# Attention of the next block set between the products of the feed forward

## The chip, the cores and the metric

The kernel runs on one core of one Trainium2 chip. Its time is device time in microseconds (us) of one execution, median of several. The engines are named PE (TensorE, matrix products; PEld is its loading of weights), DVE (VectorE), ACT (ScalarE), POOL (GpSimd) and SP (SyncE, which here only starts transfers). Each engine works through a queue of its own in order and waits on semaphores for the others.

## The reference

Three layers follow each other, all in float32.

```python
# 1: attention, batch 4, 8 heads, 576 positions, 64 wide
scores = scale * np.matmul(q, k.transpose(0, 1, 3, 2))
mask = (rel >= 0) & (rel < 64)            # a position sees itself and 63 before
attn = softmax(where(mask, scores, -1e9))
x = matmul(attn, v)                       # rearranged to (2304, 512)
# 2: feed forward, 512 -> 2048 -> 512
h = x @ w_in
g = h - np.tanh(h)
x2 = g @ w_out
# 3: eight experts, each token goes to the one with the largest cosine
logits = xn @ en.T / tau
expert_idx = np.argmax(logits, axis=1)
out[mask] = gate_w[mask, None] * (np.maximum(x2[mask] @ w1[e], 0.0) @ w2[e])
```

The products of layers 2 and 3 are made in three passes: each operand is split in a rounded part (high) and the rest (low), and high x high, high x low and low x high are added up in PSUM.

## The kernel before

**Attention** is a stage of its own at the start. Its unit of work is a *group*: for one pair of heads, three blocks of 64 positions (GB = 3). A batch has 12 groups (4 pairs of heads x 3 windows of 192 positions), so there are 48 (NG). The work on group g is spread over steps of a pipeline (`attention_step`); in step j

- PE transposes q and k of group j (`transpose_qk`, L1003), does the scores of j-1 (`score`, L1012), transposes the weights of j-5 (`transpose_p`, L1021) and multiplies those of j-7 by v (`attend`, L1032);
- DVE takes q (scaled) and k of group j out of PSUM (`evacuate`, L721 and L723), masks the scores of j-1 and finds their maximum (`mask_max`, L728), inverts the sums of j-3 (L749, L754) and copies v of group j-5 from the lower to the upper half of the partitions (`shift_v`, L738), since each block sees the one before it too;
- ACT does three exps for j-1 (`exp`, L536), copies the transposed weights of j-5 (`copy_pT`, L544) and the attended group j-7 (`copy_x`, L553, two copies of 64x192) into `xT`, which holds x of all tokens, transposed;
- POOL multiplies the weights of j-3 by the inverse sums (`normalise`, L416) and between that splits w_in (L428, L431) from a staging tile, a piece every third step;
- SP starts the loads of q, k and v, and one row block of w_in per batch.

**Feed forward** follows. A block is 384 tokens (TB), there are 6 (NBLK). For each of 16 chunks c of 128 hidden columns: PE makes the first product (12 matmuls of 384 columns, `first_product`) and the second product of chunk c-2 (9 matmuls of 512 columns, `second_product`), both through `products` (L1059 to L1061); ACT does tanh (L581), DVE h - tanh(h) (L796), ACT rounds it (L585), DVE makes its rest (L798). The second product adds up in three PSUM banks (`acc`); at c == 2 of the next block they are copied out, and at c = 3 to 11 the router of that block has its turn on PE, DVE and ACT (`after_block`: transposes of x2 at L1097, logits, choice of an expert, rank in its table); SP stores x2 and POOL scatters the slots. At c = 10 to 13 ACT and DVE split x of the next block, `xT` into `xh` and `xl` (`round_x` L571, `rest_x` L785). While the first block runs, POOL splits w_out (L478, L480), whose rows come in through the tile x2.

**Experts**: at the end the tables are planned, and 25 tiles of up to 128 tokens are gathered, put through two products with the expert's weights, and scattered. The first expert's weights are fetched once x of the last block has been split.

Both first stages run their middle part in loops with a register as counter (`attention`, `feed_forward`), with a first and a last part written out.

Of the kernel before, what the change touches and what calls it, by code (L numbers as in the profile page):

```python
# [6 lines left out]
F32R = mybir.dt.float32r  # L7
# [4 lines left out]
ds = bass.ds  # L12
# [5 lines left out]
HEAD = 9  # L18
# [16 lines left out]
def build(nc, q, k, v, w_in, w_out, emb, tau, w1, w2, out):  # L35
# [15 lines left out]
    NT = T // P  # L51

# [9 lines left out]
    with ExitStack() as ctx:  # L62
# [37 lines left out]
        changes = sb("changes", [P, NTILE + 1])  # L100

        phase1 = ctx.enter_context(ExitStack())
        xT = sb("xT", [P, NW, PAIRS, GT], scope=phase1)
        win_h = sb("win_h", [P, KC, F], F32R, phase1)
        win_l = sb("win_l", [P, KC, F], F32R, phase1)
        attn = ExitStack()

        vw = [sb(f"vw{i}", [P, NB + 1, 2, D], scope=attn) for i in range(PAIRS)]
        qbd = [sb(f"qbd{i}", [P, NB, 2, WINDOW], scope=attn) for i in range(2)]
        sm = [sb(f"sm{i}", [P, GB, P], scope=attn) for i in range(4)]  # L110
        pn = [sb(f"pn{i}", [P, GB, P], scope=attn) for i in range(4)]
# [3 lines left out]
        plain_ones = sb("plain_ones", [P, P], scope=attn)  # L115
        plain_tri = sb("plain_tri", [P, P], scope=attn)
# [5 lines left out]
        stage = sb("stage", [P, 2, F], scope=attn)  # L122

        kT = [sb(f"kT{i}", [P, NB + 1, WINDOW], scope=attn) for i in range(2)]
        qk = [sb(f"qk{i}", [P, NB, 2, D], scope=attn) for i in range(2)]
        attn.close()
        wout_h = sb("wout_h", [P, FC, DM], F32R, phase1)
        wout_l = sb("wout_l", [P, FC, DM], F32R, phase1)
        xh = sb("xh", [P, KC, 2, 2, GT], F32R, phase1)
        xl = sb("xl", [P, KC, 2, 2, GT], F32R, phase1)  # L130
        early = ExitStack()
# [3 lines left out]
        zrow = sb("zrow", [1, DM], scope=early)  # L135
        en1 = sb("en1", [E, 3], scope=early)
        enroot = sb("enroot", [E, 1], scope=early)
        early.close()
        gf_tile = sb("gf", [P, 2, TB], scope=phase1)
        gf = [gf_tile[:, i, :] for i in range(2)]  # L140
        gh = [sb(f"gh{i}", [P, TB], F32R, phase1) for i in range(2)]
        gl = [sb(f"gl{i}", [P, TB], F32R, phase1) for i in range(2)]
# [3 lines left out]
        x2T, junk = (xT[:].rearrange("p w k t -> p (w k t)")[:, i * BANK:(i + 1) * BANK] for i in (0, 1))  # L146
# [38 lines left out]
        first_loaded, v_shifted = sem("first_loaded"), sem("v_shifted")  # L185
        qk_loaded, v_loaded = sems("qk_loaded", 2), sems("v_loaded", PAIRS)
        win_loaded, win_split = sem("win_loaded"), sem("win_split")
        win_high = sem("win_high")
        qk_transposed, qk_evacuated = sem("qk_transposed"), sem("qk_evacuated")
        scored, maxed, exped = sem("scored"), sem("maxed"), sem("exped")  # L190
        sum_padded, inverted, normed = sem("sum_padded"), sem("inverted"), sem("normed")
        p_transposed, pT_copied, attended, x_copied = sem("p_transposed"), sem("pT_copied"), sem("attended"), sem("x_copied")
        wout_loaded = sems("wout_loaded", ST)
        wout_high, wout_split = sem("wout_high"), sem("wout_split")
        x_high, x_split = sem("x_high"), sem("x_split")
# [26 lines left out]
        psT, psS, psP, psO = ([grouped(2 * n + i) for i in range(2)] for n in range(4))  # L222
        psH = [banks[:, i, 0:TB] for i in (0, 1)]
        acc = [banks[:, 2 + i, :] for i in range(ST)]
        psX = banks[:, 5, :]
        psX_last = [banks[:, i, :] for i in (5, 2, 3)]
        psJ = banks[:, 0, :]
        psL = banks[:, 6, 0:ST * E].rearrange("p (s e) -> p s e", s=ST)
        psR = banks[:, 7, 0:ST * E].rearrange("p (s e) -> p s e", s=ST)
        psN = banks[:, 7, 0:E]  # L230
# [15 lines left out]
        def attention(eng, step):  # L246

            for j in range(HEAD):
                step(0, j)
            with eng.Fori(0, B - 1) as b:  # L250
                for j in range(HEAD, HEAD + GPB):
                    step(b, j)
            for j in range(HEAD, GPB + 7):
                step(B - 1, j)

        def feed_forward(eng, step):

            for c in range(FC):
                step(0, c)
            with eng.Fori(1, NBLK - 1) as n:  # L260
                for c in range(FC):
                    step(n, c)
            for c in range(FC):
                step(NBLK - 1, c)
# [28 lines left out]

        block = ctx.enter_context(nc.Block())

        @block.sync
        def _(sp):
            def load_qk(b, hp):
                i = hp % 2

                wait(sp, qk_transposed, 0 if isinstance(b, int) and PAIRS * b + hp < 2 else GPB * b + GP * (hp - 1))
                for blocks, to in ((q_blocks, qk[i][0:WINDOW]), (k_blocks, qk[i][WINDOW:P])):
                    for h in range(2):
                        sp.dma_start(to[:, :, h, :], blocks[:, ds((2 * PAIRS * b + 2 * hp + h) * NB, NB), :]).then_inc(qk_loaded[i], 16)

            def load_v(b, hp):
                if not isinstance(b, int) or b > 0:

                    sp.wait_ge(attended, GPB * b + GP * (hp + 1 - PAIRS))
                for h in range(2):  # L310
                    sp.dma_start(vw[hp][0:WINDOW, 1:, h, :], v_blocks[:, ds((2 * PAIRS * b + 2 * hp + h) * NB, NB), :]).then_inc(v_loaded[hp], 16)

            def load_w_in(row):
                sp.dma_start(stage[:, ds(row % 2, 1), :], win_rows[:, ds(row, 1), :]).then_inc(win_loaded, 16)

            def load_batch(b, more=True):

                for hp in range(PAIRS):
                    load_v(b, hp)
                    if hp + 2 < PAIRS or more:  # L320
                        load_qk(b + (hp + 2) // PAIRS, (hp + 2) % PAIRS)
                    if hp == 1 and more:

                        sp.wait_ge(win_high, 4 * b + 1)
                        wait(sp, win_split, 4 * b)
                        load_w_in(b + 1)


            for units, loaded in ((slice(0, GB), first_loaded), (slice(GB, NB), qk_loaded[0])):
                for blocks, to in ((q_blocks, qk[0][0:WINDOW]), (k_blocks, qk[0][WINDOW:P])):  # L330
                    for h in range(2):
                        sp.dma_start(to[:, units, h, :], blocks[:, h * NB + units.start:h * NB + units.stop, :]).then_inc(loaded, 16)
            load_qk(0, 1)
            load_w_in(0)
            load_batch(0)
            sp.dma_start(embs[:], emb).then_inc(small_loaded, 16)
            sp.dma_start(tau1[:], tau.rearrange("(a b) -> a b", a=1).broadcast_to((P, 1))).then_inc(small_loaded, 16)

# [3 lines left out]
            with sp.Fori(1, B - 1) as b:  # L342
                load_batch(b)
            load_batch(B - 1, more=False)


            for c in range(FC):
                wait(sp, wout_split, c - ST + 1)
                sp.dma_start(x2[:, c % ST, :], wout_rows[:, c, :]).then_inc(wout_loaded[c % ST], 16)

            def store(n):
                sp.wait_ge(acc_copied, ST * n + ST)
                sp.dma_start(x2_dram[ds(n * TB, TB), :].rearrange("(s p) n -> p s n", p=P), x2).then_inc(x2_stored, 16)
# [15 lines left out]
            with sp.Fori(0, NBLK - 1) as n:  # L369
                store(n)  # L370

            sp.wait_ge(x_split, KC * NBLK)
            fetch_w1(None, 0, None)
            fetch_w2(None, 0, None)
            store(NBLK - 1)
# [16 lines left out]
        def _(pool):  # L392
# [17 lines left out]
            pool.sem_inc(masks_made, 1)  # L410

            def normalise(b, j):
                g = GPB * b + j
                hold(pool, inverted, g + 1)
                hold(pool, p_transposed, g - 3)
                pool.tensor_tensor(pn[j % 4][:], sm[j % 4][:], rr[:, j % 4, :].unsqueeze(2).broadcast_to((P, GB, P)),  # L416
                                   ALU.mult).then_inc(normed, 1)

            def split_w_in(b, j):

                quarter = j // 3
                piece = slice(quarter * BANK, (quarter + 1) * BANK)
                raw = stage[:, ds(b % 2, 1), piece].rearrange("p k f -> p (k f)")
                high = win_h[:, ds(b, 1), piece].rearrange("p k f -> p (k f)")
                low = win_l[:, ds(b, 1), piece].rearrange("p k f -> p (k f)")
                if j % 3 == 0:
                    hold(pool, win_loaded, 16 * b + 16)
                    pool.tensor_copy(high, raw).then_inc(win_high, 1)  # L428
                elif j % 3 == 2:
                    hold(pool, win_high, 4 * b + quarter + 1)  # L430
                    pool.tensor_tensor(low, raw, high, ALU.subtract).then_inc(win_split, 1)  # L431

            for j in range(GPB):
                normalise(0, j)
                split_w_in(0, j)
                if j == 1:
                    alone(pool.memset(padrow[:, :, 0:1], float(T)))
                    alone(pool.memset(padrow[:, :, 1:2], 0.0))
                    alone(pool.memset(zrow[:], 0.0))
                    pool.sem_inc(pads_made, 1)  # L440
# [837 lines left out]
```

## Time and profile before

| | us |
|---|---|
| median of 3 runs | 901.97 (901.59 to 902.38) |
| span of the profiled execution | 897.8 |
| attention, start to the first matmul of the feed forward | 148.3 |
| feed forward | 424.5 |
| router of the last block, plan, experts | 325.0 |

The span goes from the first to the last instruction of one execution. The profile gives no other time for that execution; the runs shown lie 3.8 to 4.6 us above its span. Busy time counts an instruction from its start to its end; matmuls overlap their neighbours, so how fast PE goes is read from start to start. "Idle before" is the gap before an instruction on its engine, and behind the arrow stands what released it.

### The profile page before, as it was taken

To read this page: it belongs to the slowest core of one execution; us is meant where nothing else is said; L and a number is where in the kernel's file an instruction comes from. 1 tells how busy PE (TensorE), PEld (TensorE's weight loads), DVE (VectorE), ACT (ScalarE), POOL (GpSimd) and SP (SyncE) were. 2 spreads that over 40 slices of the span, in tenths; PEclk is the share of its full clock that TensorE was granted. 3 is DMA by queue.
4 is the path that set the end of the run, shared out by engine and by line. 5 is a ranking of instruction groups with operands and counts; after the bars stand their busy time and mean duration, and the time that the engine had idled before them with its cause. 6 is when DMAs were issued, how large, how long until landed. Compare 5 with 4: busy or idle time off the path is not lost. (4 is left out here: it accounts for less than half of the span.)

```text
span 897.8 us, 16837 instructions
## 1 busy us (share of the span) xinstructions
PE 826.8 (92%) x4496; PEld 726.4 (81%) x4497; DVE 431.8 (48%) x1214; ACT 368.3 (41%) x888; POOL 188.9 (21%) x224
## 2 busy tenths in 40 slices
PE   5988878999999999999999999758999999999992
PEld 4877777999999999999999999637888888888871
DVE  6999996332343343344334334465435152355312
ACT  3888886233222223223223222506435262455423
POOL 3755557900001001001001001021111111111111
PEclk9999999999999999999999999869999999999996
DMA  9966841300000000000000320006634251655110
GB/s 166 185 147 142 133 92 36 118 1 32 5 1 1 35 0 0 35 0 0 35 0 0 128 95 1 36 25 223 224 120 141 79 193 41 224 216 212 64 36 25
DMA packets 80463, 72.87 MB, mean 81 GB/s; under 512 B 60364, under 2 KB 60497, under 8 KB 79906
## 3 DMA queue, kind: packets, MB, share of 16 engines
q1 hardware_dynamic: 75794, 61.00, 24.3%
q0 software_dynamic: 4624, 11.32, 3.9%
q8 instruction: 22, 0.36, 0.2%
q14 instruction: 23, 0.19, 0.1%
HBM read 138.19 MB, written 11.44 MB: 167 GB/s over the span
## 5 line engine op out<-in xcount | busy, mean ns | idle before, releaser
L1059 PE MATMUL banks<-xh,win_h 128*128 (+1 forms) x384 | 132.5, 345 | 0.0
L1061 PE MATMUL banks<-xh,win_l 128*128 (+1 forms) x384 | 129.4, 337 | 0.0
L1060 PE MATMUL banks<-xl,win_h 128*128 (+1 forms) x384 | 129.1, 336 | 0.0
L798 DVE TENSOR_TENSOR gl<-gf,gh 128x384 fp32r<-128x384 f32 x96 | 56.3, 587 | 145.2 <-ACT gh L585 145.2
L1061 PE MATMUL banks<-wout_h,gl 128*128 128x512 f32 x288 | 113.9, 395 | 0.0
L1060 PE MATMUL banks<-wout_l,gh 128*128 128x512 f32 x288 | 113.7, 395 | 0.0
L585 ACT CAST gh<-gf 128x384 fp32r<-128x384 f32 x96 | 49.3, 514 | 153.2 <-PE banks L1061 152.0
L1059 PE MATMUL banks<-wout_h,gh 128*128 128x512 f32 x288 | 112.2, 389 | 0.0
L796 DVE TENSOR_TENSOR gf<-banks,gf 128x384 f32<-128x384 f32 x96 | 53.4, 557 | 114.3 <-ACT gf L581 114.3
L581 ACT ACTIVATE gf<-banks 128x384 f32<-128x384 f32 x96 | 47.2, 492 | 148.3 <-PE banks L1061 148.3
L961 DVE TENSOR_TENSOR hTl<-banks,hTh 128x512 fp32r<-128x512 f32 x50 | 32.3, 686 | 92.4 <-ACT hTh L669 92.3
L1059 PEld LDWEIGHTS banks<-xh,win_h 128*128 128x128 f32 x384 | 72.2, 188 | 2.6
L1060 PEld LDWEIGHTS banks<-xl,win_h 128*128 128x128 f32 x384 | 72.2, 188 | 2.5
L1059 PE MATMUL banks<-w1h,xgh 128*128 x176 | 70.5, 400 | 2.7 <-DVE xgl L969 2.7
L1061 PEld LDWEIGHTS banks<-xh,win_l 128*128 128x128 f32 x384 | 72.0, 188 | 0.0
L1059 PE MATMUL banks<-w2h,hTh 128*128 x176 | 70.8, 402 | 0.9 <-DVE hTl L961 0.9
L536 ACT ACTIVATE sm<-sm,nmx 128x128 f32<-128x128 f32 x144 | 56.2, 391 | 33.5 <-DVE nmx L728 33.5
L1061 PE MATMUL banks<-w2h,hTl 128*128 x176 | 68.9, 392 | 0.0
L1061 PE MATMUL banks<-w1h,xgl 128*128 x176 | 68.8, 391 | 0.0
L1060 PE MATMUL banks<-w1l,xgh 128*128 x176 | 68.7, 390 | 0.0
L1060 PE MATMUL banks<-w2l,hTh 128*128 x176 | 68.6, 390 | 0.0
L484 POOL TENSOR_TENSOR norm<-ss,power 128x3 f32<-128x3 f32 x6 | 5.3, 884 | 297.5 <-DVE ss L819 281.0
(181 smaller groups left out, 1532.0 us busy)
## 6 DMA issues: line engine op xcount, KB each, us to landing
w1raw<-in_moe_w_dram SPq DMA_DIRECT2D x104, 512.0 KB
w2raw<-in_moe_w_dram SPq DMA_DIRECT2D x104, 512.0 KB
vw<-in_v_dram SPq DMA_DIRECT2D x32, 144.0 KB, 4.0
x_rows<-x SPq DMA_DIRECT2D x6, 768.0 KB, 3.6
qk<-in_q_dram SPq DMA_DIRECT2D x30, 144.0 KB, 3.2
qk<-in_k_dram SPq DMA_DIRECT2D x30, 144.0 KB, 3.6
stage<-in_moe_w_in_dram SPq DMA_DIRECT2D x4, 1024.0 KB, 6.4
x<-in_moe_w_out_dram SPq DMA_DIRECT2D x16, 256.0 KB, 2.6
```

The source lines that it names most:

```text
L484: pool.tensor_tensor(norm[:], ss[:], power[:], ALU.pow).then_inc(rooted, 1)
L536: last = act.activation(sm[j % 4][:, u, :], sm[j % 4][:, u, :], ACT.Exp, bias=nmx[:, j % 4, u:u + 1], scale=-1.0, accum_out=rs[:, j % 4, u ...
L581: act.activation(gf[c % 2][:], psH[c % 2], ACT.Tanh).then_inc(tanh_ready, 1)
L585: act.copy(gh[c % 2][:], gf[c % 2][:]).then_inc(g_high, 1)
L796: dve.tensor_tensor(gf[c % 2][:], psH[c % 2], gf[c % 2][:], ALU.subtract).then_inc(g_ready, 1)
L798: dve.tensor_tensor(gl[c % 2][:], gf[c % 2][:], gh[c % 2][:], ALU.subtract).then_inc(g_split, 1)
L961: dve.tensor_tensor(hTl[:, part, :], psHT[half].rearrange("p (k t) -> p k t", k=KC), hTh[:, part, :], ALU.subtract).then_inc(hT_split, 1)
L1059: pe.matmul(to, sh, mh, start=start, stop=False)
L1060: pe.matmul(to, sh, ml, start=False, stop=False)
L1061: return pe.matmul(to, sl, mh, start=False, stop=stop)
```

## The change

Only the attention of the first block (8 groups: 4 pairs of heads x 2 windows of 192) still runs ahead of the feed forward. The groups are renumbered so that 8 in a row make up one block (`FIRST`). The other 40 are set between the products. Each of the 16 steps of a block has two half steps (`SLOTS` = 32 in a block): one after the first product, one after the second. A table gives each group the half step in which it begins, every third one in block 0, every fourth from then on; its other pieces follow 1 to 8 half steps later on each engine. All loops are written out.

- The attended group goes no more to `xT`: ACT copies it from PSUM in rounded form into `xh`, DVE subtracts that from PSUM and writes `xl`. `xT`, `round_x` and `rest_x` are gone.
- v is loaded twice, to the upper half and, one block of 64 earlier, to the lower; `shift_v` is gone. Keys are kept per pair of heads (`kT`), with the last 64 columns of the window before carried over by DVE.
- The scaled weights are written over the unscaled ones (`pn` is gone).
- PSUM: in the feed forward one bank serves both transposed q, k and scores, another both transposed weights and attended values. The router is left with one bank: x2 is transposed by halves of two 128-column pieces, copied in six parts in place of three.
- w_in and w_out come whole into tiles of their own, in column pieces and row pieces; POOL splits w_in by 128 columns, two pieces ahead of the first product that uses them, the first block's step by step; w_out is rounded by ACT and its rest made by DVE, one chunk in each step of block 0, in place of POOL.
- Fetching the first expert's weights waits for the last attended group; the store of block 4 is issued behind it.

The diff, cut to its core (PE's new order, the half steps, and the pieces of each engine):

```diff
-HEAD = 9
+LAG_SCORE, LAG_TURN, LAG_ATTEND = 1, 6, 7
+    FIRST, SLOTS = 2 * PAIRS, 2 * FC
+        def psT(g):
+            return grouped((5, 0)[g % 2] if g < FIRST else 5)
+        def psS(g):
+            return grouped((1, 2)[g % 2] if g < FIRST else 5)
+        def psP(g):
+            return grouped((6, 3)[g % 2] if g < FIRST else 6)
+        def psO(g):
+            return grouped((7, 4)[g % 2] if g < FIRST else 6)
...
+        def first_slot(g):
+            n, i = g // FIRST - 1, g % FIRST
+            return 3 * i if n == 0 else SLOTS * n + 4 * i - 8
+        begins = {first_slot(g): g for g in range(FIRST, NG)}
+        def begun(s, lag):
+            return begins.get(s - lag)
...
+        def steps(n):
+            for c in range(FC):
+                yield c, SLOTS * n + 2 * c
...
@@ sync
+            load_qk(0, (0, GB))
+            load_qk(0, (GB, 2 * GB))
+            load_qk(1)
+            load_v(0)
+            load_v(1)
+            load_win(0)
+            load_qk(2)
+            load_qk(3)
+            load_v(2)
+            load_wout(0)
+            load_qk(4)
+            load_v(3)
+            load_win(1)
+            load_wout(1)
...
+            sp.wait_ge(attended, NG)
+            sp.wait_ge(table_cleared, 32)
             fetch_w1(None, 0, None)
             fetch_w2(None, 0, None)
+            store(NBLK - 2)
             store(NBLK - 1)
...
@@ gpsimd
+            constants(0)
+            for j in range(FIRST + 5):
+                if 3 <= j < FIRST + 3:
+                    normalise(j - 3)
+                if j in (4, 5):
+                    split_w_in(j - 4)
+            def pieces(s):
+                if (g := begun(s, 3)) is not None:
+                    normalise(g)
+            for n in range(NBLK):
+                for c, s in steps(n):
+                    if n == 0 and c + 2 < FC:
+                        split_w_in(c + 2)
+                    pieces(s)
+                    pieces(s + 1)
...
@@ scalar
+            def copy_x(g):
+                n, kk, a = g // FIRST, pair_of(g), g % 2
                 act.wait_ge(attended, g + 1)
+                wait(act, h_ready, FC * (n - 1))
                 for h in range(2):
                     rows = slice(h * D, (h + 1) * D)
+                    last = act.copy(xh[rows, kk, n % 2, a, :].rearrange("p (g c) -> p g c", g=GB),
+                                    psO(g)[rows, :, h * WINDOW:(h + 1) * WINDOW])
                 last.then_inc(x_copied, 1)
+            for j in range(FIRST + 5):
+                if 1 <= j < FIRST + 1:
+                    exp(j - 1)
+                if 4 <= j < FIRST + 4:
+                    copy_pT(j - 4)
+                if 5 <= j:
+                    copy_x(j - 5)
+            def pieces(s):
+                if (g := begun(s, 2)) is not None:
+                    exp(g)
+                if (g := begun(s, LAG_TURN)) is not None:
+                    copy_pT(g)
+                if (g := begun(s, LAG_ATTEND)) is not None:
+                    copy_x(g)
...
+                    tanh(n, c)
+                    pieces(s)
+                    high_g(n, c)
+                    pieces(s + 1)
+                    if n == 0:
+                        high_w_out(c)
...
@@ vector
+            def evacuate(g):
+                i, hp = g % 2, pair_of(g)
                 dve.wait_ge(qk_transposed, g + 1)
+                wait(dve, scored, g - 1)
                 for h in range(2):
                     rows = slice(h * D, (h + 1) * D)
+                    dve.tensor_scalar(qbd[i][rows, :, h, :], psT(g)[rows, :, 0:WINDOW], float(D) ** -0.5, None, ALU.mult)
+                wait(dve, scored, g if g % 2 else g - FIRST + 2)
+                if window_of(g) % GP:
+                    carries[0] += 1
+                    dve.tensor_copy(kT[hp][:, 0, :], kT[hp][:, GB, :]).then_inc(carried, 1)
+                    dve.wait_ge(carried, carries[0])
+                dve.tensor_copy(kT[hp][:, 1:1 + GB, :], psT(g)[:, :, WINDOW:P]).then_inc(qk_evacuated, 1)
+            def split_x(g):
+                n, kk, a = g // FIRST, pair_of(g), g % 2
+                dve.wait_ge(x_copied, g + 1)
+                for h in range(2):
+                    rows = slice(h * D, (h + 1) * D)
+                    high, low = (x[rows, kk, n % 2, a, :].rearrange("p (g c) -> p g c", g=GB) for x in (xh, xl))
+                    last = dve.tensor_tensor(low, psO(g)[rows, :, h * WINDOW:(h + 1) * WINDOW], high, ALU.subtract)
+                last.then_inc(x_split, 1)
+            for j in range(FIRST + 6):
+                if j >= 6:
+                    split_x(j - 6)
+                if j < FIRST:
+                    evacuate(j)
...
+            def pieces(s):
+                if (g := begun(s, LAG_ATTEND + 1)) is not None:
+                    split_x(g)
+                if (g := begun(s, 0)) is not None:
+                    evacuate(g)
+                if (g := begun(s, 3)) is not None:
+                    pad_sum(g)
+                    invert(g)
+                if (g := begun(s, LAG_SCORE)) is not None:
+                    dve.wait_ge(scored, g + 1)
+                    dve.wait_ge(p_transposed, g - 3)
+                    mask_max(g, [0, 1, 2])
...
+            for n in range(NBLK):
+                for c, s in steps(n):
+                    if n > 0 and c == 2:
+                        copy_acc(n - 1)
+                    less_tanh(n, c)
+                    pieces(s)
+                    if n > 0 and c in (4, 6, 8):
+                        square(n - 1, (c - 4) // 2)
+                    if n > 0 and c == 10:
+                        choose(n - 1)
+                    if n > 0 and c == 12:
+                        place(n - 1)
+                    low_g(n, c)
+                    pieces(s + 1)
+                    if n > 0 and 3 <= c < 3 + 2 * ST:
+                        copy_x2T(n - 1, c - 3)
+                    if n == 0:
+                        low_w_out(c)
...
@@ tensor
+            for j in range(FIRST + 5):
+                if j < FIRST:
+                    transpose_qk(j)
+                if 1 <= j < FIRST + 1:
+                    score(j - 1)
+                if 4 <= j < FIRST + 4:
+                    transpose_p(j - 4)
+                if 5 <= j:
+                    attend(j - 5)
+            def pieces(s):
+                if (g := begun(s, LAG_ATTEND)) is not None:
+                    attend(g)
+                if (g := begun(s, LAG_TURN)) is not None:
+                    transpose_p(g)
+                if (g := begun(s, LAG_SCORE)) is not None:
+                    score(g)
+                if (g := begun(s, 0)) is not None:
+                    transpose_qk(g)
...
+            for n in range(NBLK):
+                for c, s in steps(n):
+                    first_product(n, c)
+                    pieces(s)
+                    if c >= 2:
+                        second_product(n, c - 2)
+                    elif n > 0:
+                        second_product(n - 1, c + FC - 2)
+                    pieces(s + 1)
+                    if n > 0:
+                        route(n - 1, c)
+                    if n == 0 and c == 8:
+                        transpose_emb()
```

## Rows read from the trace of the kernel before

**Rows 1.** The page's busy table: busy us, share of the span, instructions.

```profile
PE 826.8 (92%) x4496; PEld 726.4 (81%) x4497; DVE 431.8 (48%) x1214; ACT 368.3 (41%) x888; POOL 188.9 (21%) x224
```

**Rows 2.** Busy time by stage: stretch, length, busy us of each engine, PE's clock, DMA.

```profile
148.30:572.80 424.50, 424.46 (x2218) 385.47 (x2217) 156.99 (x378) 113.42 (x231) 52.26 (x52) 1.00 0.08 28
0.00:148.30 148.30, 113.86 (x868) 102.26 (x869) 135.61 (x595) 111.91 (x438) 80.41 (x118) 0.99 0.68 131
572.80:897.80 325.00, 288.47 (x1412) 238.66 (x1412) 139.16 (x241) 142.94 (x219) 56.26 (x55) 0.94 0.37 128
```

**Rows 3.** Waits of the first 150 us: us in total, times, longest.

```profile
PE banks L1012 <- DVE kT L723: 19.4, 38, 1.3
```

**Rows 4.** Timeline of PE, attention: start, us, instruction, number, idle before.

```profile
20.41 0.55 PE L1003 MATMUL banks<-ident,qk 128*128 128x128 f32 x3 [2.66 <-DMA qk<-in_k_dram]
...
25.43 0.49 PE L1003 MATMUL banks<-ident,qk 128*128 128x128 f32 x3
...
27.43 0.49 PE L1003 MATMUL banks<-ident,qk 128*128 128x128 f32 x3
...
63.06 0.94 PE L1012 MATMUL banks<-kT,qbd 128*128 128x128 f32 x6 [0.41 <-DVE kT L723]
```

**Rows 5.** Timeline of DVE, attention.

```profile
61.06 0.82 DVE L738 COPY vw<-vw 64x384 f32<-64x384 f32 x1
61.91 0.72 DVE L721 TENSOR_SCALAR qbd<-banks 64x192 f32<-64x192 f32 x2
62.65 0.36 DVE L723 COPY kT<-banks 128x192 f32<-128x192 f32 x1
...
64.65 0.72 DVE L721 TENSOR_SCALAR qbd<-banks 64x192 f32<-64x192 f32 x2
```

**Rows 6.** Timeline of ACT, attention.

```profile
61.06 0.40 ACT L536 ACTIVATE sm<-sm,nmx 128x128 f32<-128x128 f32 x1 [0.43 <-DVE nmx L728]
...
62.35 0.48 ACT L544 COPY pT<-banks 128x384 f32<-128x384 f32 x1
62.73 0.64 ACT L553 COPY xT<-banks 64x192 f32 x2
```

**Rows 7.** Timeline of PE, feed forward.

```profile
237.65 0.60 PE L1097 MATMUL banks<-ident,x 128*128 128x128 f32 x4
238.00 0.42 PE L1059 MATMUL banks<-xh,win_h 128*128 x1
238.26 0.34 PE L1060 MATMUL banks<-xl,win_h 128*128 x1
...
240.20 0.39 PE L1059 MATMUL banks<-wout_h,gh 128*128 128x512 f32 x1
...
242.28 0.95 PE L1107 MATMUL banks<-enT,xT 128*128 128x8 f32 x8
```

**Rows 8.** Timelines of ACT and DVE, feed forward.

```profile
240.40 0.49 ACT L581 ACTIVATE gf<-banks 128x384 f32<-128x384 f32 x1 [1.98 <-PE banks L1061]
...
240.92 0.56 DVE L796 TENSOR_TENSOR gf<-banks,gf 128x384 f32<-128x384 f32 x1 [1.31 <-ACT gf L581]
```

**Rows 9.** Timeline of SP's queue, two transfers started.

```profile
11.36 1.28 SPq L304 DMA_DIRECT2D qk<-in_q_dram  x2
```

**Rows 10.** The page's DMA issues: number, KB each, median us to landing.

```profile
qk<-in_k_dram SPq DMA_DIRECT2D x30, 144.0 KB, 3.6
```

**Rows 11.** Groups by line: number, busy us, mean ns.

```profile
L431 POOL TENSOR_TENSOR win_l<-stage,win_h (+1 forms) x16 | 22.0, 1376 | 0.0
L428 POOL CAST win_h<-stage (+1 forms) x16 | 11.7, 732 | 0.0
```

**Rows 12.** Timeline of PE after the wait for the expert tables.

```profile
593.30 4.21 PE L1154 MATMUL banks<-w1h,ones 128*128 128x512 f32 x9
```

More of the change, by code:

```diff
@@ L313, in load_w_in @@
[L313 to L326, printed above, removed]
@@ L329, in _, with parts @@
[L329 to L335, printed above, removed]
+            def parts(u):
+                n = u // PAIRS
+                one, two = 2 * n, 2 * n + 1
+                if one // GP == two // GP:
+                    return ((one, 0, 2 * GB),)
+                return (one, 0, GB), (two, GB, 2 * GB)
@@ new lines, in load_qk @@
+            def load_qk(u, only=None):
+                wait(sp, qk_transposed, 2 * u - 2)
+                for w, start, end in parts(u):
+                    if only is not None:
+                        start, end = only
+                    for blocks, to in ((q_blocks, qk[u % 2][0:WINDOW]), (k_blocks, qk[u % 2][WINDOW:P])):
+                        for h in range(2):
+                            at = (2 * PAIRS * (w // GP) + 2 * (u % PAIRS) + h) * NB + GB * (w % GP) + (start if only else 0)
+                            loaded = first_loaded if only and start == 0 else qk_loaded[u % 2]
+                            sp.dma_start(to[:, start:end, h, :], blocks[:, at:at + end - start, :]).then_inc(loaded, 16)
@@ L341, in _ @@
             sp.dma_start(x2_dram[T:T + 1, :], zrow[:]).then_inc(table_cleared, 16)
[L342 to L353, printed above, removed]
+            for s in range(SLOTS * (NBLK - 1)):
+                turned, left = begun(s, 0), begun(s, LAG_ATTEND)
+                if turned is not None and turned % 2 == 1 and turned // 2 + 2 < NG // 2:
+                    load_qk(turned // 2 + 2)
+                if left is not None and left % 2 == 1 and left // 2 + 2 < NG // 2:
+                    load_v(left // 2 + 2)
+                if s >= SLOTS and s % SLOTS == 7:
+                    store(s // SLOTS - 1)
             def fetch_w1(s, e, changed):
@@ L1006, in score, with loads @@
-            def score(b, j):
-                g = GPB * b + j
-                i, first = j // GP % 2, j % GP * GB
-                pe.wait_ge(qk_evacuated, g + 1)
-                wait(pe, maxed, g - 1)
-                for u in range(first, first + GB):
-                    last = pe.matmul(psS[j % 2][:, u - first, :], qbd[i][:, u, :, :].rearrange("p h c -> p (h c)"), kT[i][:, u:u + 2, :],
+            def loads(u, each):
+                n = sum(each * (1 if v // PAIRS % GP != 1 else 2) for v in range(u % 2, u + 1, 2))
+                return 16 * n
@@ new lines, in transpose_x2 @@
+            def transpose_x2(m, i):
+                st, half = i // 2, i % 2
+                pe.wait_ge(acc_copied, ST * m + ST)
+                wait(pe, x2T_copied, 2 * ST * m + i)
+                wait(pe, slotted, m)
+                if m == 0 and i == 0:
+                    pe.wait_ge(en_ready, 1)
+                for kk in range(2):
+                    at = (2 * half + kk) * P
+                    last = pe.transpose(psX[:, kk * P:(kk + 1) * P], x2[:, st, at:at + P], ident[:])
+                last.then_inc(x2_transposed, 1)
```

643 lines of the change are left out of this document (291 added, 352 removed).

## The prediction

> **What bounds the kernel now.** I read the page's busy table first: PE (TensorE) is busy for 92% of the span, DVE (VectorE) for 48% [rows 1]. A share over the whole span hides stages, so I then cut the span at the first and the last matmul of the feed forward (FF) [rows 2]. In the attention stage, 148.3 us, PE is busy for 113.9 and DVE for 135.6. In the FF stage, 424.5 us, PE is never idle and DVE works 157.0. In the experts' stage, 325 us, the change touches little. The waits of the first stage say the same: PE's matmuls for the scores waited 38 times, 19.4 us in all, for the key copy on DVE [rows 3].
>
> So attention is bound by DVE and the FF by PE. One group of attention takes DVE 2.74 us in steady state, 61.91 to 64.65 [rows 5]. Where PE has no wait it takes 2.00 us, 25.43 to 27.43 [rows 4]. The most that moving attention under the FF can save is what DVE costs beyond PE; PE's own work does not get cheaper, it moves from a stage where it was 77% busy to one where it is the bound.
>
> **The change part by part.**
>
> *Removed:* the attention stage ahead of the first FF matmul, 148.3 us [rows 2].
>
> *Added first: a shorter stage for the first block's 8 groups.* It costs more per group than before. Issues: SP sends 12 query and key transfers, 8 of v (now loaded twice), one of w_in and then the 4 for groups 4 and 5; 25 issues at 0.64 us [rows 9] from 0.8 us end near 17 us, and landing takes 3.6 us more [rows 10]: group 4 starts at about 21 us. (Before, the wait of this kind came at group 6, until 20.41 [rows 4].) Then a step of DVE is 2.74, less the v copy with its gap (61.06 to 61.91, 0.85), plus the new subtraction and a carried key column. The subtraction is twice 64x192 from PSUM, which has no row. Bounds: 0.36 each like the 64x192 scaling [rows 5] and 0.56 each like the 128x384 subtraction [rows 8]. I take 0.36, since 192 columns go through in both; 0.72 in all. The carry (128x64, two groups of three, with a wait of DVE on itself) has no row either: between nothing and the 0.36 of the 128x192 copy [rows 5], taken as 0.2. Step: 2.74 - 0.85 + 0.72 + 0.15 = 2.8.
> By the Trainium skill (VectorE: DVE Perf Modes, the table of PSUM to SBUF costs) such an operation costs 120 cycles plus its columns at 0.96 GHz; by that estimate it is 0.33, and the stall worked out below would be 0.65 in place of 0.7.
> From step 6 DVE begins each step with the subtraction of group j-6, and waits there for ACT's copy of the same group. ACT does that copy only after the three exps of group j-2, which wait for the masks that DVE has just ended: from the first exp to the end of the copy it is 61.06 to 63.37, 2.3 us [rows 6]. DVE and ACT thus take turns in steps 6, 7 and 8, 5.2 us each. Group 4 at 21, group 5 at 23.8, end of masks 25.4, and three steps of 5.2 give 41; the last exps end at 42. Then group 7 still goes through inversion, scaling on POOL, transposition, copy, product, copy and subtraction with the others queued in front of it, about 8 us. First FF matmul: 51. Bounds: 46 (loads no later than before) to 58 (v loads of groups 6 and 7, issued only when group 3 is attended, late too).
>
> *Added second: PE's work for 40 groups inside the FF.* At least 2.00 us per group. Between FF products each visit has a price when PE returns: after 4 transposes (237.65 to 238.00) the second FF matmul comes 0.26 us after the first, where the other eleven up to 240.20 take 0.18 each [rows 7]. So 0.09 per visit, four visits, less what is hidden (3 transposes are then 0.26 and not the 0.33 of [rows 4]): 2 x 0.35 + 2 x 0.76 = 2.22, times 40 = 89. Bounds 80 (no price) and 100 (each visit with the 0.94 of a score after a wait).
>
> *Added third: a wait of PE for DVE in the second half of each step with a new group.* PE transposes q and k behind a first product, does a second product, and then the scores, which need q and k from DVE. PE is back after 0.35 + 0.09 + 2.08 = 2.5 us [rows 7]. On DVE, counted from the same point (240.20): tanh on ACT ends at 240.89, DVE's subtraction starts at 240.92 and lets the next operation in about 0.48 later, at 1.2 [rows 8]. Then stand the subtraction of the group before (0.72) and the scaling and copy of the new one, 61.91 to the score's 63.06, 1.15 [rows 4, 5], and in two of three groups the carry, 0.2. Sum 1.2 + 0.72 + 1.15 + 0.15 = 3.2. PE stalls 0.7. DVE's queue is in order, so nothing lets the copy pass. From block 1's first groups on all begin at an even half step, 4 apart, and the subtraction (8 after the start) meets the start of a later one: 30 of 40 groups have this clash, 30 x 0.7 = 21. The groups of block 0 are 3 apart and miss it; 2.5 against 2.5 there, I take nothing. Bounds 0 and 33 (0.56 per subtraction).
> Queued behind the stalled score on PE is all that follows, the next first product included, so the stall is paid in full.
>
> *Further waits.* The product with v needs the copy of the turned weights, which on ACT stands behind tanh and three exps: 0.2 + 0.49 + 1.29 + 0.48 = 2.45 [rows 6, 8], against PE's 2.5: taken as 0.05 for 32 groups. In the steps that also hold the router's chains on DVE (2 of 16) mask and copy come later: 0.5 each. With the splits of w_in on POOL and w_out on ACT and DVE, 5 us in all, bounds 0 and 15. POOL has 1.4 + 0.7 for one piece of w_in [rows 11] in a step of over 5 us, so it hides; w_out on ACT and DVE at about 0.6 each hides as well, each engine being under 4 us of a step.
>
> *Moved:* x2 is transposed by 2 x 128 columns: 3 more returns of PE per block, 1 us over 5 blocks. w1 is still fetched when attention is over, at the end of block 4, and the store of block 4 goes behind these 8 transfers; nothing waits for it until block 5 ends. Experts' stage: 0 (-2 to +4).
>
> *Sum:* 897.8 - 148.3 + 51 + 89 + 21 + 5 + 1 = 916.5 span. The median of the runs shown is 902.0, 4.2 above this execution's span; with the same on top: 921 us.
>
> **The rivals.**
> *A, all waits hide (faster).* If DVE's copy of the keys reaches the score within 2.5 us of the first product's end, the sum is 897.8 - 148.3 + 49 + 87 + 1 + 4.2 = 891. It decides at 0.05 us per group: with 51, 89, 5 and 1, only 1.5 us may be left of the 21. For it: DVE has 60% of each step free, and 0.7 is a difference of two sums. Against: each term of the 3.2 is a row or close to one, and the order is fixed.
> *B, more than one stall per group.* ACT's and DVE's queues hold the pieces of two groups in order; one late piece (mask behind the low part of g, exps ahead of the high part) makes a second stall of about 0.7 to 1. 40 more of these give 950. Against: apart from the two named, each hand-over has a product of 2.1 us as slack.
> *C, loads.* Until 35 us some 5 MB are wanted, and small packets slowed SP's queue before. If w_in or v comes 8 us late: 929.
> *D, the clock.* In the short first stage PE works 2 of 5 us. At 593 us nine matmuls after an idle stretch took 4.21 us, 0.47 each, PE's lower level of 1.2 GHz [rows 12]; over the attention stage the clock was 0.99 with PE 77% busy [rows 2]. If PE leaves the first stage at the lower level, its first FF products take double, 2 to 4 us; 925.
> The Trainium skill (TensorE: Matmul & The Clock Gate, the warm-up mystery) has the throttled state as the default, which activity releases; by that rule D's 2 to 4 us would be paid, by the attention stage's row they would not.
>
> **How the numbers follow.** Forecast 0.50 (its own range 908 to 935), A 0.22, B 0.15, C 0.08, D 0.05. Low end: A with a little of the waits, 893; high end: forecast with a part of B, 940. 0.2% (1.8 us) is about what a measurement of this kernel can tell from no change. Faster by more than that are A's cases but for few: 0.20; within it 0.04; slower 0.76.
>
> **What would show it.** First FF matmul at 51 (46 to 58), and DVE idle before the new subtraction in steps 6 to 8. FF stage, first to last matmul, 541 us. PE idle before the scores, released by the key copy on DVE, 0.7 each some 30 times in blocks 1 to 4 (and at block 0's end) and hardly in block 0's first 8. PE's clock 1.00 in the FF. From the FF's last matmul to the end 325. The forecast is wrong if the PE is idle for less than 5 us in the FF (A), or if the score is not the line with most idle time (B).

## The result, and the profile after

| | before | after |
|---|---|---|
| median | 902.17 us (901.59 to 903.31, 4 runs) | 918.88 us (917.31 to 920.27, 4 runs) |
| ratio | | 1.0186, 95% interval 1.0166 to 1.0206 |
| span of the profiled execution | 897.8 | 916.4 (this execution took 918.2) |
| first FF matmul starts | 148.3 | 52.4 |
| FF, first to last matmul | 424.5 | 540.1 |
| rest | 325.0 | 323.9 |

The changed kernel is slower by 1.9%. The page's busy table of the changed kernel, which answers to [rows 1], hardly differs, so a look at it alone tells nothing:

```profile
PE 831.7 (91%) x4496; PEld 725.7 (79%) x4497; DVE 432.5 (47%) x1301; ACT 362.6 (40%) x880; POOL 156.4 (17%) x192
```

Busy time by stage, for [rows 2]. In the FF stage PE is now idle for 539.6 - 513.8 = 25.8 us, where it was never idle, and DVE's work there has grown from 157 to 269 us:

```profile
0.00:52.40 52.40, 30.01 (x144) 26.51 (x145) 23.86 (x117) 19.59 (x74) 18.89 (x39) 0.87 0.56 133
52.40:592.00 539.60, 513.80 (x2939) 460.75 (x2940) 269.23 (x943) 199.52 (x587) 81.40 (x98) 1.00 0.21 53
592.00:916.00 324.00, 287.92 (x1415) 238.41 (x1413) 139.44 (x241) 143.50 (x220) 56.14 (x55) 0.95 0.38 129
```

PE's waits between 52.4 and 592 us (total, times, longest). One line holds nearly all of it, and it is the one of [rows 3], moved. The third line ends with the first FF matmul at 52.42 and so lies ahead of the stage; the other two make up the 25.8 us:

```profile
PE banks L1109 <- DVE kT L789: 24.2, 32, 2.1
PE banks L1120 <- DVE xl L813: 1.6, 2, 1.0
PE banks L1159 <- DVE xl L813: 1.5, 1, 1.5
```

The same place on PE, for [rows 7]: behind a first product the transposes of q and k (L1100), a second product, the scores (L1109) and the next first product; the last line is the transposes of the next group, 11.39 us after those of this one:

```profile
311.46 0.49 PE L1100 MATMUL banks<-ident,qk 128*128 128x128 f32 x3
311.71 0.47 PE L1159 MATMUL banks<-wout_h,gh 128*128 128x512 f32 x1
312.02 0.39 PE L1160 MATMUL banks<-wout_l,gh 128*128 128x512 f32 x1
...
313.64 0.40 PE L1161 MATMUL banks<-wout_h,gl 128*128 128x512 f32 x1
314.79 0.94 PE L1109 MATMUL banks<-kT,qbd 128*128 128x128 f32 x6 [0.75 <-DVE kT L789]
315.48 0.42 PE L1159 MATMUL banks<-xh,win_h 128*128 128x384 f32 x1
...
322.85 0.49 PE L1100 MATMUL banks<-ident,qk 128*128 128x128 f32 x3
```

And on DVE, for [rows 5, 8]. The chain of the prediction can be read off: tanh(h) subtracted, the attended group before (L813), q scaled (L783), the carried column (L787), the keys (L789). They end 3.27 us after 311.46:

```profile
312.18 0.56 DVE L867 TENSOR_TENSOR gf<-banks,gf 128x384 f32<-128x384 f32 x1 [2.30 <-ACT gf L636]
312.66 0.71 DVE L813 TENSOR_TENSOR xl<-banks,xh 64x192 fp32r<-64x192 f32 x2
313.40 0.72 DVE L783 TENSOR_SCALAR qbd<-banks 64x192 f32<-64x192 f32 x2
314.14 0.20 DVE L787 COPY kT<-kT 128x64 f32<-128x64 f32 x1
314.37 0.36 DVE L789 COPY kT<-banks 128x192 f32<-128x192 f32 x1
```

The stage ahead of the FF, on DVE: each step starts with a wait of over 2 us for ACT's copy of the attended group. From 29.41 the steps are 5.1 and 5.2 us apart, the third is 4.1:

```profile
21.43 0.72 DVE L783 TENSOR_SCALAR qbd<-banks 64x192 f32<-64x192 f32 x2 [5.03 <-PE banks L1100]
...
29.41 0.72 DVE L813 TENSOR_TENSOR xl<-banks,xh 64x192 fp32r<-64x192 f32 x2 [2.23 <-ACT xh L607]
...
34.52 0.72 DVE L813 TENSOR_TENSOR xl<-banks,xh 64x192 fp32r<-64x192 f32 x2 [2.37 <-ACT xh L607]
...
39.73 0.72 DVE L813 TENSOR_TENSOR xl<-banks,xh 64x192 fp32r<-64x192 f32 x2 [2.37 <-ACT xh L607]
...
43.84 0.72 DVE L813 TENSOR_TENSOR xl<-banks,xh 64x192 fp32r<-64x192 f32 x2 [2.37 <-ACT xh L607]
```

### The profile page after: what moved, and what is told of

It is laid out like the page before. It is cut to its first block and busy times, and to the rows that moved or that the text cites. A ratio compares the mean times of both kernels' runs of the same rounds, so it can differ in the third digit from the quotient of the medians.

```text
span 916.4 us, 16016 instructions
## 1 busy us (share of the span) xinstructions
PE 831.7 (91%) x4496; PEld 725.7 (79%) x4497; DVE 432.5 (47%) x1301; ACT 362.6 (40%) x880; POOL 156.4 (17%) x192
## 5 line engine op out<-in xcount | busy, mean ns | idle before, releaser
L1159 PE MATMUL banks<-xh,win_h 128*128 128x384 f32 x384 | 136.5, 355 | 1.5 <-DVE xl L813 1.5
L1161 PE MATMUL banks<-xh,win_l 128*128 128x384 f32 x384 | 129.8, 338 | 0.0
L1160 PE MATMUL banks<-xl,win_h 128*128 128x384 f32 x384 | 129.3, 337 | 0.0
L1159 PE MATMUL banks<-wout_h,gh 128*128 128x512 f32 x288 | 119.1, 414 | 0.0
L469 POOL TENSOR_TENSOR sm<-sm,rr 128x384 f32<-128x384 f32 x48 | 41.7, 869 | 380.7 <-DVE rr L805 380.7
L1109 PEld LDWEIGHTS banks<-kT,qbd 128*128 128x128 f32 x288 | 40.4, 211 | 40.3 <-DVE kT L789 40.2
L1109 PE MATMUL banks<-kT,qbd 128*128 128x128 f32 x288 | 48.2, 309 | 26.3 <-DVE kT L789 26.3
```

The source lines that it names most:

```text
L469: pool.tensor_tensor(sm[g % 4][:], sm[g % 4][:], rr[:, g % 4, :].unsqueeze(2).broadcast_to((P, GB, P)), ALU.mult).then_inc(normed, 1)
L1109: last = pe.matmul(psS(g)[:, u, :], qbd[i][:, u, :, :].rearrange("p h c -> p (h c)"), kT[hp][:, u:u + 2, :], start=True, stop=True)
L1159: pe.matmul(to, sh, mh, start=start, stop=False)
L1160: pe.matmul(to, sh, ml, start=False, stop=False)
L1161: return pe.matmul(to, sl, mh, start=False, stop=stop)
```

## The experiments

All times are medians; in the sessions the kernel before ran at 901.1, 900.8 and 900.7 us.

**1. Keys ahead of the subtraction.**

```diff
             def pieces(s):              # DVE
-                if (g := begun(s, LAG_ATTEND + 1)) is not None:
-                    split_x(g)
                 if (g := begun(s, 0)) is not None:
                     evacuate(g)
+                if (g := begun(s, LAG_ATTEND + 1)) is not None:
+                    split_x(g)
```

> In the feed forward DVE takes q and k of the new group out of PSUM before it makes the rest of the attended group before, not after; nothing else differs. My theory (the scores wait because the subtraction stands ahead of the key copy in DVE's queue): the wait of the scores in blocks 1 to 4 falls from 0.75 us to under 0.1, 22 to 25 us go out of the feed forward, time about 896. Rival (the scores wait for the whole chain of tanh, DVE and the shared PSUM bank, whichever piece comes first): under 5 us go, 914 to 919.

Measured: 897.80 us (896.19 to 898.87), ratio to before 0.9958 (0.9942 to 0.9975); span 897.0, 19.4 less than the changed kernel's; FF stage 520.8, 19.3 less. PE's waits in it:

```profile
PE banks L1109 <- DVE kT L789: 3.4, 2, 2.1
```

The 24.2 us of this line have become 3.4, two waits in block 0. Two instructions of 0.36 us stood in the wrong place; nothing else changed, so the rival with the shared bank falls. The size is 19 and not 22 to 25. Where DVE has a carried column the scores still start 0.16 us late (at 305.56 in its trace; the second product's last three matmuls start 0.23 us apart from 304.71 on, so they were due at 305.40), too short to be counted as idle: some 3 us in 20 groups. And PE now waits 1.1 us in the FF for the copy of the turned weights on ACT. This alone turns the change from slower to slightly faster.

**2. Scores one half step later.**

```diff
-LAG_SCORE, LAG_TURN, LAG_ATTEND = 1, 6, 7
+LAG_SCORE, LAG_TURN, LAG_ATTEND = 2, 6, 7
-                if (g := begun(s, 2)) is not None:      # ACT: exp(g)
+                if (g := begun(s, 3)) is not None:
-                if (g := begun(s, 3)) is not None:      # DVE: sums; POOL: scaling
+                if (g := begun(s, 4)) is not None:
```

> The scores of a group inside the feed forward come one half step later, and mask, exps, inversion and scaling with them; DVE keeps its order. A first product of 2.1 us then lies between. My theory: DVE's 3.2 us are hidden wholly, no wait of PE for the key copy in blocks 1 to 4, 28 us less, about 891, a little below the kernel with the order swapped. If a late piece further on (exps, turned weights) then makes PE wait for ACT instead, as a rival has it, the saving is under 15 us and PE's idle time shows at the product with v.

Measured: 897.40 us (896.15 to 899.81), ratio 0.9964 (0.9951 to 0.9976); span 894.6, FF stage 518.8, 21.3 less than the changed kernel's. Two of PE's waits in it are new:

```profile
PE banks L1100 <- DVE nmx L794: 2.9, 2, 2.6
PE banks L1159 <- ACT x L650: 2.1, 4, 0.7
```

The wait for the keys is gone from the list. From the transposes of one group to those of the next, four half steps on, it takes 10.42 us (300.79 to 311.21) against 11.39 (311.46 to 322.85) in the changed kernel. The edit does one thing more than its text says: from block 1 on the scores of one group now fall in the half step in which the weights of an earlier one are transposed, so that PE leaves the products three times per group and not four. I expected 28 us and got 21: new waits came in block 0 (transposes of q and k for the mask of the group before, which shares their bank) and at a block's start (for ACT's copy of the FF result). The rival's mark, a wait at the product with v, does not show inside the FF.

**3. The subtraction twice.**

```diff
                 for h in range(2):      # split_x
+                    if again:           # in the feed forward, g < NG - 2
+                        dve.tensor_tensor(spare[rows, :]..., psO(g)[...], high, ALU.subtract)
                     last = dve.tensor_tensor(low, psO(g)[...], high, ALU.subtract)
```

> DVE makes each subtraction of an attended group inside the feed forward twice (once to a spare tile, two more instructions of 0.36 us), for 38 of the 40 groups. My theory: DVE's work is on the path where it stands ahead of the key copy, so each of some 30 groups pays 0.72 us, 20 to 22 us more, about 940. Rival (DVE has 50% of its time free, the wait comes from elsewhere): within 3 us of the changed kernel.

Measured: 937.76 us (936.11 to 938.72), ratio 1.0401 (1.0384 to 1.0419); span 936.9, 20.5 more than the changed kernel's, as expected. The wait grew with it:

```profile
PE banks L1113 <- DVE kT L790: 40.2, 32, 2.1
PE banks L1124 <- DVE xl L817: 3.7, 6, 1.6
```

With 0, 1 and 2 subtractions ahead of the keys the span is 897.0, 916.4 and 936.9: 19 to 20 us for each, about 0.7 us in some 28 groups.

**4. The first stage: subtraction last.**

```diff
             for j in range(FIRST + 6):   # DVE
-                if j >= 6:
-                    split_x(j - 6)
                 if j < FIRST:
                     evacuate(j)
...
                 if masks:
                     mask_max(j - 1, [1, 2])
+                if j >= 6:
+                    split_x(j - 6)
```

> In the stage ahead of the feed forward DVE makes the rest of group j-6 at the end of its step j and not at its head. My theory (DVE and ACT take turns in steps 6, 7 and 8 because the subtraction at the head waits for ACT's copy): 2.3 us go in each of these steps, the first product starts at 46 in place of 52.4, about 912.5. Rival (ACT's queue of exps and copies bounds these steps anyway): under 2 us, 917 or more.

Measured: 915.39 us (913.90 to 916.82), ratio 1.0161 (1.0144 to 1.0179); the first FF matmul at 48.4. Four of the six or seven expected microseconds; the next limit shows in PE's waits:

```profile
PE banks L1132 <- DMA vw<-in_v_dram: 4.2, 1, 4.2
```

DVE and ACT no longer took turns, and then PE waited for v of groups 6 and 7, until 43.97. Behind that wait and one of 1.5 us, PE began the FF at the lower of its two clock levels (1.2 GHz): the granted clock was 0.50 from 48.36 to 51, and the twelve matmuls of the first product were 0.32 us apart and took 4.00 us where the changed kernel's took 2.22:

```profile
48.84 0.52 PE L1160 MATMUL banks<-xl,win_h 128*128 128x384 f32 x1
49.16 0.52 PE L1161 MATMUL banks<-xh,win_l 128*128 128x384 f32 x1
```

**5. Experiments 1 and 4 with SP's loads reordered.**

```diff
             load_v(0)
+            load_qk(2)
             load_v(1)
             load_win(0)
-            load_qk(2)
             load_qk(3)
             load_v(2)
+            load_v(3)
             load_wout(0)
             load_qk(4)
-            load_v(3)
```

> Keys before the subtraction in the feed forward; in the first stage the subtraction at the end of DVE's step, and SP's loads reordered (q and k of groups 4 and 5 before v of groups 2 and 3, v of groups 6 and 7 before the first part of w_out and the next q and k). My theory: the start is bound by DVE and ACT taking turns and by the loads of v and q, k; both gone, the first product starts at about 44 in place of 52.4 (48.4 with the subtraction moved alone), time 889. Rival (the memory bandwidth of the first 50 us, not the order, sets it): start at 48 or later, 893.

Measured: 886.08 us (884.02 to 890.55), ratio 0.9845 (0.9805 to 0.9885); first FF matmul at 41.0, FF stage 518.1. The bytes are the same, so the order of the loads set the start and the rival (bandwidth) falls. It was worth 7.4 us beyond experiment 4; experiment 8, with the same first stage, starts the FF at 42.7, so 5.7 to 7.4 is what the traces support.

**6. The kernel before, v loaded twice.**

```diff
                 for h in range(2):      # load_v, before.py
                     sp.dma_start(vw[hp][0:WINDOW, 1:, h, :], ...).then_inc(v_loaded[hp], 16)
+                    sp.dma_start(vw[hp][WINDOW:P, 0:NB, h, :], ...).then_inc(v_loaded[hp], 16)
...
-                if whole >= 5 and whole - 5 < NG:
-                    shift_v(b, j - 5)   # DVE
```

PE's product with v waits for the loads in place of the copy.

> The kernel before, with v loaded a second time to the upper half and DVE's copy of v left out; nothing of attention moved. My theory (attention was bound by DVE's 2.74 us per group, 0.85 of them that copy): the group then takes ACT's 2.35 us, the stage ends near 131 in place of 148.3, time 885, below all kernels with attention moved so far. Rival (the transfers bind: 4.7 MB more in the same stretch, near 210 GB/s): under 8 us gained, 894 or more.

Measured: 893.08 us (891.90 to 898.93), ratio 0.9924 (0.9901 to 0.9948); the FF starts at 140.2. Faster, but only by half of what I expected: 7.7 us, at the edge of the rival's range (under 8 us gained, 894 or more).

**7. PE's product with v twice**, on experiment 2's kernel.

```diff
-                for v in range(GB):     # attend
+                for v in tuple(range(GB)) * (1 if g < FIRST else 2):
```

> The kernel with later scores, where PE makes the 6 matmuls with v of each of the 40 groups in the feed forward a second time. My theory (with no wait left, each microsecond of PE's attention work is paid in full): 40 x 0.58 = 23 us more than that kernel, 919 to 921. Rival (some of PE's work still hides in waits for ACT and DVE or behind weight loading): under 15 us more.

Measured: 919.71 us (916.85 to 920.73), ratio 1.0196 (1.0167 to 1.0226); FF stage 542.3, 23.5 more than in experiment 2, where 40 x 0.58 = 23.2 were expected (by the medians 22.3). This part of PE's attention work in the FF is paid in full; the rival (under 15) falls.

**8. Everything together.** Edits of 1, 2 and 4 with the loads of 5.

> All of it: scores one half step later, keys before the subtraction, subtraction last in the first stage, loads reordered. My theory: the two cures of the wait share one gain, so the feed forward is that of the kernel with later scores (518.8 us) and the start 44 to 46: 887 to 889, at most 2 us below the kernel with keys first and the short start. Rival (they add up): 870.

Measured: 885.21 us (884.17 to 886.85), ratio 0.9820 (0.9796 to 0.9845), level with experiment 5: the two cures take away the same wait. Busy time by stage:

```profile
0.00:42.60 42.60, 25.73 (x144) 22.99 (x145) 23.98 (x117) 19.60 (x74) 15.20 (x35) 0.88 0.45 114
42.60:561.40 518.80, 511.22 (x2940) 462.06 (x2940) 281.71 (x944) 199.11 (x587) 93.88 (x102) 1.00 0.23 59
```

**9. Two visits per group.** Experiment 8 with LAG_ATTEND 8 for 7, and in the FF DVE's subtraction again ahead of the keys, as in the changed kernel.

> The kernel with all cures, but the product with v one half step later too (and the subtraction behind it, before the keys again, which it no longer meets): PE then leaves the feed forward's products twice per group and not three times. Theory: each return costs 0.08 us, so 40 x 0.08 = 3 us less than the kernel with all cures, about 882. Rival (waits at the shared bank for weights and attended values, whose order is now tight in block 0, take it back): 885 or more.

Measured: 906.74 us (904.90 to 908.94), ratio 1.0068 (1.0051 to 1.0085), 21.5 more than experiment 8. A miss, and the rival's case:

```profile
PE banks L1120 <- DVE xl L813: 23.7, 15, 2.3
```

Turned weights and attended values share a bank, so the transposes of group g wait for the subtraction of g-1. The groups of block 0 are three half steps apart, and there both now fall in the same half step: eight waits of about 2 us each up to 145 us, 16.1 us in all, such as

```profile
91.17 0.52 PE L1120 MATMUL banks<-ident,sm 128*128 128x128 f32 x3 [2.26 <-DVE xl L813]
```

From then on the subtraction stands one half step ahead in place of two, and PE waits only now and then, 7.6 us in seven waits. At 301 us the chain for the expert choice stands ahead of it on DVE, and PE waits 1.3 us until 302.37:

```profile
300.93 0.18 DVE L914 TENSOR_TENSOR onehot<-em,r 128x24 fp32r<-128x24 f32 x1
301.03 0.55 DVE L871 TENSOR_TENSOR gl<-gf,gh 128x384 fp32r<-128x384 f32 x1
301.50 0.72 DVE L813 TENSOR_TENSOR xl<-banks,xh 64x192 fp32r<-64x192 f32 x2
```

What a return costs was thus not measured by itself.

**10. Experiment 6 without the added transfers of batches 1 to 3.** The upper half of v keeps the first batch's values, so the kernel leaves out the right values of v there; the work of the engines is the same.

```diff
+                    if isinstance(b, int) and b == 0:
                         sp.dma_start(vw[hp][WINDOW:P, 0:NB, h, :], ...)    # as in 6
```

> The kernel before without DVE's copy of v, and with the second load of v left out from the second batch on: the upper half of v keeps the first batch's values, so the attention of three batches is computed with wrong values of v there. It tells what held the kernel with v loaded twice. Theory: the transfers did (PE waited 19.7 us for q and k). Without them the feed forward starts at 131 to 133 in place of 140.2, time 885. Rival (ACT with 2.35 us per group did, busy 19.5 of 20 us in some stretches): 138 or later, 891 or more.

Measured: 889.62 us (886.91 to 891.54), ratio 0.9873 (0.9850 to 0.9896); the FF starts at 137.5, between both expectations. PE's waits for q and k are 14.8 us here and 19.7 in experiment 6:

```profile
PE banks L1002 <- DMA qk<-in_k_dram: 14.8, 4, 5.2
```

So the added transfers of three batches cost 2.7 us of stage 1. Those of the first batch are still in, and all of the 14.8 us lie in the first 39 us, where the kernel before waits 10.6. SP, with the added starts of v in front, had started the q and k of group 12 by 34.8 and not by 30.8 us, and PE transposes that group 3.6 us later (first line: the kernel before, second: this one):

```profile
35.16 0.55 PE L1003 MATMUL banks<-ident,qk 128*128 128x128 f32 x3 [0.32 <-DMA qk<-in_k_dram]
38.79 0.55 PE L1002 MATMUL banks<-ident,qk 128*128 128x128 f32 x3 [2.72 <-DMA qk<-in_k_dram]
```

From there to the first FF matmul it takes 98.7 us here and 113.1 in the kernel before: 14.4 less in 36 groups, 0.40 for each. The pace in the middle, some 7.0 us for three groups by the spacing of SP's loads, is ACT's 2.35, and 2.74 less 2.35 is 0.39. The theory holds where no load is waited for; of its 17 us the first 12 groups, which run at the pace of the loads, gave nothing and lost 3.6. No run separates the first batch's transfers from the rest.

## Why the prediction was right

The forecast was 921, the sum of the span 916.5; measured were 918.9 and 916.4. Most of the 2 us between forecast and median is the difference of a median and a span, taken as 4.2 and found to be 2.5. Step by step:

- *The shorter first stage, 51 (46 to 58)*: 52.4. Group 4 was transposed at 20.5 (21 forecast), the waits for ACT's copy came where they were put, the last exps ended at 42.8 (42). Inside this two errors cancelled: the masks that end the fifth step were done at 27.2 and not at 25.4, and the three steps took 5.0, 5.2 and 4.1 and not 5.2 each, the last having no new q and k. The tail took 9.6; the text says 8 and its total of 51 has room for 9. Experiment 4 confirms the turns DVE and ACT took. It also shows the loads of v of groups 6 and 7, which the prediction had in its upper bound of 58, close behind as the next limit (experiment 5).
- *PE's work for 40 groups, 89 (2.22 each)*: slightly high. From start to start q and k take 0.25, the scores 0.69, the weights 0.24, v 0.58, and each return 0.08 to 0.09: 2.10, or 84 us. The largest part of the difference is v, taken at 0.67. Experiment 7 shows for v that it is paid one for one.
- *The wait before the scores, 0.7 in 30 groups, 21*: mechanism, place and number of groups right. The trace shows 24.2 us idle in 32 waits, 30 of them (20.8 us) behind block 0's first groups. Idle time understates what is lost: one group follows the other 11.39 us later with the carried column and 11.15 without (217.04 to 228.19), against 10.5 without wait, 0.9 and 0.65. That is some 24.5 in 30 groups rather than 21. At 311.46 DVE takes 3.27 us (3.2 forecast) and PE's work meanwhile 2.41 (2.5). Experiments 1 and 3 take the cause away and double it.
- *Further waits, 5*: 5.0 us idle, but by luck, since they are not the ones named. PE did not wait before the product with v. In their place stood the scores of the first two groups of block 0 (2.1 and 1.3 us), which have no second product ahead of them because its first two steps have none, and two waits for the subtraction (1.6 us). The prediction had taken nothing for block 0's scores.
- *Experts' stage 0*: 323.9 for 325.0.
- *The price of a subtraction*, for which there was no row: 0.35 each (L813, the mean of 96), as taken from the 64x192 scaling. The Trainium skill's table (VectorE: DVE Perf Modes, the table of PSUM to SBUF costs) gave 0.33 by estimate; the measurement decides. A formula below that table, 151 cycles plus the columns at 0.96 GHz, gives 0.36 by estimate.

That the sum came within 0.1 us is luck: 5 us too much for PE's work stood against 3.5 too little for the keys, 1.4 too little for the first stage and 1.5 us of lower clock (below) that no term held. One sum in the text does not follow from its terms: rival A leaves 1.5 us of the 21 for waits, but 897.8 less the 895.5 of the other terms is 2.3.

The rivals: A needed DVE's keys within 2.5 us and they came at 3.3; but experiment 1 shows how near it was, one exchange of two calls away. B's second stall per group did not come here; experiment 9 has stalls of that kind, for the shared bank, 15 of them. C did not happen in the changed kernel; experiments 4 and 5 show how little room the loads had. D did not happen as stated: the first product in the FF ran at a granted clock of 1.00. But behind the idle 2.08 us before block 0's first scores the clock was 0.51 and then 0.50 from 57.2 to 60.5, the lower level (1.2 GHz). The scores took 1.30 us in place of 0.69, and half of chunk 1's first product ran 0.32 us apart in place of 0.18, about 1.5 us in all:

```profile
57.20 1.65 PE L1109 MATMUL banks<-kT,qbd 128*128 128x128 f32 x6 [2.08 <-DVE kT L789]
...
58.97 0.52 PE L1160 MATMUL banks<-xl,win_h 128*128 128x384 f32 x1
59.29 0.52 PE L1161 MATMUL banks<-xh,win_l 128*128 128x384 f32 x1
```

By the Trainium skill (TensorE: Matmul & The Clock Gate, the warm-up mystery) the throttled state is the default and activity releases it; the trace agrees in kind, and in experiment 4 D came as stated, at 1.8 us.

Where the hoped-for gain went: a group cost 2.74 us on DVE and costs 2.10 on PE, so moving 40 could win 25.6 us. The first stage gave 13.7 of these back: 148.3 less 40 x 2.74 would have been 38.7, and it took 52.4. The FF grew by 115.6 us: 84 for PE's work, 24.5 for the keys in blocks 1 to 4, and 7.1 more, which the 5.0 of other idle time, the 1.5 of lower clock and the router's added returns (1 by forecast, not measured) account for within half a microsecond. 1.1 came out of the rest: in all 18.6, the difference of the spans. With the start shortened to 41 and the wait gone, the same idea gives 886 and 885.

## What to carry to other kernels

When work is moved under an engine that is already the bound, only what the old place cost beyond that engine's own work can be won; write that difference down first. Then follow each hand-over through the in-order queue of the other engine with durations and compare it with what the bound engine does meanwhile: here 3.3 us against 2.4 decided the sign, and swapping two calls decided it the other way. A bank shared by two uses turns a change of order elsewhere into a wait; a free slot in the schedule is only free if the bank is.

## What the runs showed beyond that

- The order in which SP starts its loads was worth 5.7 to 7.4 us in the first 50 (first FF matmul at 48.4 in experiment 4, at 42.7 and 41.0 in 8 and 5), with the same bytes.
- Doubling v's transfers in three of the four batches of the kernel before cost 2.7 us, though the DMA engines moved 182 to 208 GB/s between 20 and 120 us (experiment 6). In the first batch it made PE wait 3.6 us longer for the q and k of group 12.
- A matmul waiting for a semaphore starts later than its idle time tells: at 314.79 the trace counts 0.75 us idle, but the next matmul would have been due at 313.87, 0.92 earlier, since matmuls start 0.23 us apart here and are shown 0.40 long. Waits are better priced by the spacing of starts.
